# A routing tail reordered: pad addresses ahead of places, five pad scatters behind the first rows' low part, fewer filler matmuls

## The reference

```python
def reference(**kw):                                     # B, H, S, D = 4, 8, 768, 48
    attn_out = _attn_ref(r, k, v, w, u)                  # decayed linear attention, per head 48 x 48 state
    x = attn_out.transpose(0, 2, 1, 3).reshape(3072, 384)
    gate = 1.0 / (1.0 + np.exp(-(x @ w_gate)))           # 384 -> 1536
    x = gate * (x @ w_val) @ w_out                       # 1536 -> 384
    xn, en = x / (norm(x) + 1e-6), emb / (norm(emb) + 1e-6)
    logits = xn @ en.T / tau                             # 8 experts
    expert_idx = np.argmax(logits, axis=1)
    gate_w = softmax(logits)[np.arange(N), expert_idx]
    for e in range(8):
        mask = expert_idx == e
        out[mask] = gate_w[mask, None] * (np.maximum(x[mask] @ w1[e], 0.0) @ w2[e])   # 384 -> 1024 -> 384
    return out
```

## Time and profile before

| | |
|---|---|
| runs | 866.97 us median, 865.52 to 870.53 |
| profiled execution | 868.17 us, its span 866.4 us |
| PE busy | 835.3 us, 96% of the span |
| DVE, ACT, POOL busy | 448.5, 297.5, 415.4 us |
| mean granted TensorE clock | 0.976 |
| DMA | 82.02 MB, mean 95 GB/s |

### The profile page before, as it was taken

The page is one execution under the profiler, slowest core; times in us unless marked ns, Lnnn a source line. Parts: engine busy times, 40 slices in busy tenths (PEclk is TensorE's granted clock), DMA queues, the critical chain, the costliest instruction groups (busy, mean ns, idle before and its releaser), DMA issues.

```text
span 866.4 us, 20325 instructions
## 1 busy us (share of the span) xinstructions
PE 835.3 (96%) x7442; PEld 789.6 (91%) x7443; DVE 448.5 (52%) x1057; ACT 297.5 (34%) x610; POOL 415.4 (48%) x446
## 2 busy tenths in 40 slices
PE   5999899999999999999999999989999999999995
PEld 5899899999999999999999999978999999989995
DVE  7579555455455455355455451485267277267100
ACT  1134322322232232232232233514444544444442
POOL 4346245435436436426427413254566566466444
PEclk8599999999999999999999999999999999999999
DMA  9643413203202302302302200236345344344110
GB/s 281 219 125 123 132 35 97 68 29 87 85 28 85 86 26 79 95 20 85 95 19 86 88 20 10 74 128 178 96 140 161 100 146 147 107 155 142 45 36 29
DMA packets 78420, 82.02 MB, mean 95 GB/s; under 512 B 5816, under 2 KB 75648, under 8 KB 78352
## 3 DMA queue, kind: packets, MB, share of 16 engines
q1 hardware_dynamic: 65200, 60.29, 23.2%
q10 hardware_dynamic: 9216, 9.55, 3.8%
q0 software_dynamic: 3936, 11.23, 3.5%
HBM read 69.83 MB, written 12.01 MB: 94 GB/s over the span
## 4 chain that ended last, share of the span: by engine, by line
PE 93%; DVE 4%; issue 1%; POOL 1%; DMA 0%; ACT 0%; SPq 0%; POOLq 0%; ACTq 0%; DVEq 0%
PE ps L1340 34%; PE ps L1361 18%; PE ps L1443 14%; PE ps L1428 13%; PE ps L1451 3%; PE ps L1286 2%; PE ps L1263 2%; PE ps L1383 2%; PE ps L1294 1%; PE ps L1270 1%; PE ps L1300 1%; PE ps L1408 1%; DVE weights L1125 1%; PE ps L1310 1%; DMA w_col<-in_w 0%
## 5 line engine op out<-in xcount | busy, mean ns | idle before, releaser
L1340 PE MATMUL ps<-x_groups,weights 128*128 128x384 f32 x1728 | 319.5, 341 | 0.2 <-DVE weights L1125 0.2
L1340 PEld LDWEIGHTS ps<-x_groups,weights 128*128 128x128 f32 x1728 | 301.1, 190 | 2.6 <-issue 0.5
L614 POOL TENSOR_TENSOR hT<-gate,hT 128x384 fp32r<-128x384 f32 x96 | 104.5, 1091 | 144.7 <-ACT hT L743 144.7
L1361 PE MATMUL ps<-weights,hT 128*128 128x392 f32 x864 | 160.6, 344 | 0.0
L1361 PEld LDWEIGHTS ps<-weights,hT 128*128 128x128 f32 x864 | 152.6, 188 | 0.4
L1443 PE MATMUL ps<-weights,hT 128*128 x672 | 124.2, 339 | 1.7 <-ACT h_f L851 1.7
L1428 PE MATMUL ps<-weights,x_groups 128*128 (+1 forms) x504 | 122.8, 397 | 1.2 <-issue 1.2
L1082 DVE TENSOR_TENSOR gate<-ps,gate 128x384 f32<-128x384 f32 x96 | 53.5, 557 | 126.3 <-PE ps L1340 119.7
L1443 PEld LDWEIGHTS ps<-weights,hT 128*128 128x128 f32 x672 | 115.9, 188 | 1.9 <-issue 1.9
L1428 PEld LDWEIGHTS ps<-weights,x_groups 128*128 128x128 f32 x504 | 92.6, 188 | 20.4 <-issue 1.7
L1068 DVE CAST weights<-staged 128x768 fp32r<-128x768 f32 x56 | 49.0, 874 | 93.1 <-PE ps L1428 54.8
(11 more groups left out here) (179 smaller groups left out, 970.7 us busy)
## 6 DMA issues: line engine op xcount, KB each, us to landing
staged<-in_moe_w SPq DMA_DIRECT2D x60, 384.0 KB
r_in<-routed ACTq DMA_DIRECT2D x30, 192.5 KB
rk_raw<-in_rt SPq DMA_DIRECT2D x21, 256.0 KB, 3.6
rk_raw<-in_kt SPq DMA_DIRECT2D x21, 256.0 KB, 4.1
r_in<-in_r SPq DMA_DIRECT2D x21, 192.0 KB, 2.4
k_in<-in_k SPq DMA_DIRECT2D x21, 192.0 KB, 2.5
v_in<-in_v SPq DMA_DIRECT2D x21, 192.0 KB, 2.3
A_room<-in_v_swap SPq DMA_DIRECT2D x21, 96.0 KB, 2.7
```

What stands on the lines that cost most here:

```text
L614: g.tensor_tensor(hT_lo[:, f, :], gate[:, f % 2, :], hT_hi[:, f, :].bitcast(F32), ALU.subtract).then_inc(hlo_ready, 1)
L1340: ins = te.matmul(ps[:, bank[f % 2], 0:GT], wt[:, c, fs], x[:, half, c, :], start=(c == 0 and m == 0), stop=(c == KC - 1 and m == 2))
L1361: ins = te.matmul(ps[:, BX2[i], 0:XW], h[:, f, ts], wt[:, f, :], start=(f == 0 and m == 0), stop=(f == FC - 1 and m == 2))
```

## The change

It does four things. In `weigh` two small DVE instructions (the cast of the token number and its increment) now stand that stood in `scale`; in `scale` the token's copy into the row comes first and the scaled row last, with `rows_ready` on it, and `choose` waits for that. In `put` of the last tile the two instructions that make the pads' addresses come before those that make the rows' places. On POOL pads 2 to 5 go from before `keep_tokens(0)` and `rows_lo(0)` to behind them, in front of pads 6 and 7 (five pads, 2 to 6, count to `pads_out`, as before). On PE the fillers go from 36 and 14 to 32 and 4.

```diff
--- before.py
+++ after.py
@@ -655,8 +655,6 @@
                 pad(0, first_pad)
                 scatter(G, half, 2)
                 pad(1, second_pad)
-                for e in range(2, E - 2):
-                    pad(e, pads_out)
 
             for i in range(TPG):
                 for stage in range(STAGES):
@@ -709,7 +707,8 @@
 
             keep_tokens(0)
             rows_lo(0)
-            pad(E - 2, pads_out)
+            for e in range(2, E - 1):
+                pad(e, pads_out)
 
             pad(E - 1, stored)
             def finish(last):
@@ -999,6 +998,8 @@
                 T = G * TPG + i
                 logits = x2[:, DM:XW]
                 dve.wait_ge(x2_psum, T + 1)
+                if T > 0:
+                    dve.wait_ge(rows_ready, T)
                 ve.tensor_copy(x2[:, :], ps[:, BX2[i], 0:XW]).then_inc(x2_copied, 1)
                 dve.wait_ge(x2_copied, T + 2)
                 ve.tensor_reduce(top[:, i, 0:1], logits, AX_X, ALU.max).then_inc(route_step, 1)
@@ -1020,24 +1021,28 @@
                 dve.wait_ge(route_step, T * 9 + 5)
                 ve.scalar_tensor_tensor(out=top[:, i, 4:5], in0=top[:, i, 0:1], scalar=-1.0, in1=top[:, i, 3:4],
                                         op0=ALU.mult, op1=ALU.mult).then_inc(bias_ready, 1)
+                ve.tensor_copy(token_i[:, :], token[:, :]).then_inc(route_step, 1)
+                dve.wait_ge(route_step, T * 9 + 6)
+                ve.tensor_scalar(token[:, :], token[:, :], float(P), None, ALU.add).then_inc(route_step, 1)
 
             def scale(G, half, i):
 
                 T = G * TPG + i
                 buf = (half * TPG + i) % 2
+                dve.wait_ge(route_step, T * 9 + 7)
+                ve.tensor_copy(row[:, buf, DM:ROW].bitcast(I32), token_i[:, :])
                 dve.wait_ge(probs_ready, T + 1)
                 ve.tensor_scalar(top[:, i, 5:6], top[:, i, 5:6], 1e-9, None, ALU.add).then_inc(route_step, 1)
-                dve.wait_ge(route_step, T * 9 + 6)
+                dve.wait_ge(route_step, T * 9 + 8)
                 ve.reciprocal(top[:, i, 6:7], top[:, i, 5:6]).then_inc(route_step, 1)
-                dve.wait_ge(route_step, T * 9 + 7)
-                ve.tensor_scalar(row[:, buf, 0:DM], x2[:, 0:DM], top[:, i, 6:7], None, ALU.mult)
-                ve.tensor_copy(token_i[:, :], token[:, :]).then_inc(route_step, 1)
-                dve.wait_ge(route_step, T * 9 + 8)
-                ve.tensor_copy(row[:, buf, DM:ROW].bitcast(I32), token_i[:, :])
-                ve.tensor_scalar(token[:, :], token[:, :], float(P), None, ALU.add).then_inc(route_step, 1)
-
                 dve.wait_ge(route_step, T * 9 + 9)
-                dve.sem_inc(rows_ready, 1)
+                ve.tensor_scalar(row[:, buf, 0:DM], x2[:, 0:DM], top[:, i, 6:7], None, ALU.mult).then_inc(rows_ready, 1)
+
+            def pads():
+
+                ve.tensor_scalar(pad_at[:, :], filled[:, :], lane[:, 0:1], None, ALU.add).then_inc(pad_step, 1)
+                dve.wait_ge(pad_step, 1)
+                ve.tensor_copy(pad_i[:, :], pad_at[:, :]).then_inc(pads_ready, 1)
 
             def put(b, G, half, i):
 
@@ -1050,6 +1055,8 @@
                 ve.tensor_tensor(place_m[:, :], place[:, :], chosen[:, i, :], ALU.mult).then_inc(place_step, 1)
                 ve.tensor_tensor(filled[:, :], ranks[:, E:2 * E], filled[:, :], ALU.add).then_inc(place_step, 1)
                 dve.wait_ge(place_step, T * 4 + 3)
+                if T == NT - 1:
+                    pads()
                 ve.tensor_reduce(pos[:, buf, :], place_m[:, :], AX_X, ALU.add).then_inc(place_step, 1)
                 dve.wait_ge(place_step, T * 4 + 4)
                 dve.wait_ge(scattered[buf], (b * TPG + ((half * TPG + i) // 2 + 1)) * 16)
@@ -1112,11 +1119,6 @@
                     put(b, G, half, 2)
                 else:
                     put(b, G, half, 2)
-
-                    dve.wait_ge(place_step, (G * TPG + 2) * 4 + 3)
-                    ve.tensor_scalar(pad_at[:, :], filled[:, :], lane[:, 0:1], None, ALU.add).then_inc(pad_step, 1)
-                    dve.wait_ge(pad_step, 1)
-                    ve.tensor_copy(pad_i[:, :], pad_at[:, :]).then_inc(pads_ready, 1)
                     scale(G, half, 2)
 
             def make_lo(kind, j):
@@ -1461,9 +1463,9 @@
                 if first:
                     pe.wait_ge(plan, 4)
 
-            keep_clock(BT, 36)
+            keep_clock(BT, 32)
             turn_rows(0)
-            keep_clock(BT, 14)
+            keep_clock(BT, 4)
             run_slots(pe, slot, output)
```

## The result

The changed kernel takes 873.31 us (median of 7 runs, 872.47 to 875.72); the kernel before, on the same chip, 868.87 us (7 runs, 865.52 to 870.53). The ratio is 1.0064, 95% interval 1.0052 to 1.0076: slower by more than the 0.5% that a measurement of this kernel can tell from no change. The forecast was 867.2 in a range of 864.6 to 869.8.

A forecast was written before the change was run, and what follows sets the result against it. PE, holding 93% of the chain, was taken to bound the kernel, measured at slot 0's output start. Terms of -0.1 and +0.3 for the clock summed to +0.2, giving 867.2 us on the median, range 864.6 to 869.8.

The forecast's parts named there:

- the moved pads: POOL, behind slot 0's low part: six pads instead of two delay load 2, so output starts at 599.5, before 599.60.
- A: Start of ACT's first copy of slot 0's rows after the transposes: from 585.22 to 583.6, bounds 584.9 and 582.0.
- rival (a): The gain gets through if the 1.39 before ACT's copy was pad traffic: output at 597.2, 864.6 us; chance 0.22 with (e).
- The last pad's landing: Before ACT's load 2: landing 1.85 later by the quiet row, more beside traffic; load 2 at A + 11.6 to 12.5.
- Load 2's flight and what follows: From load 2 to slot 0's output: flight 3.0 to 4.26, then transposes 0.33; output at A + 14.9 to 17.1.
- The clock: PE's new pauses inside `hidden(1)` and before slot 2's rows may lower the clock: bounds 0 and 1.6, 0.3 taken.
- The fillers: PE around slot 0's transposes: with 8 records left behind them, `hidden(0)` starts at 584.1 instead of 587.99, 3.9 us earlier.
- the point by which I measured: Start of slot 0's output matmuls on PE, 599.60 before; every us it moves moves the end by one us.
- Rival (b): The moved pads cost more than the earlier start brings: output at 600.9, 868.3 us, 869.9 with low clock; chance 0.12.
- (c): Fewer fillers and PE's two new pauses lower the clock in the output matmuls: 1.6 instead of 0.3, 868.5 us; chance 0.08.
- (d): The pads delay expert 1's weights so that PE waits for them: a few us, 872 and more; chance 0.03.
- (e): Only the fillers act and the pads hide: `hidden(0)` and all behind it 2.4 earlier, 864.6 us; chance 0.22 with (a).

The follow-up runs named there:

- experiment 9: The changed kernel with expert 1's weight loads held back until all pads have landed; 870.57 us against 867.16 for the kernel before, ratio 1.0036.
- experiment 4: The changed kernel with the old 36 and 14 fillers; 872.9 us against 867.69 for the kernel before, ratio 1.0066.
- experiment 12: The changed kernel with slot 1 written out on PE and 16 fillers in the wait for load 2; 872.53 us against 866.44 for the kernel before, ratio 1.0071.
- experiment 3: The kernel before with only the fillers changed, 32 and 4 instead of 36 and 14; 867.58 us against 867.69, ratio 0.9999.
- experiment 5: The changed kernel with load 2 waiting for pad 2 alone, pads 3 to 6 awaited before load 3; 868.98 us against 865.35 before, ratio 1.0043.
- experiment 7: The kernel of experiment 6 with fillers 10 and 1 of 512 columns for 32 and 4 of 128; 868.92 us against 865.35 before, ratio 1.0044.
- experiment 6: The changed kernel with load 2 waiting for pad 2 alone and pads 5 to 7 behind slot 1's low part; 866.57 us against 865.35, ratio 1.0000.
- experiment 8: The changed kernel with pads 2 and 3 put back ahead of the first rows; 871.78 us against 865.35 for the kernel before, ratio 1.0073.
- experiment 1: The changed kernel with pads 2 to 5 put back ahead of the first rows; 867.76 us against 867.69 for the kernel before, ratio 0.9995.
- experiment 10: The kernel of experiment 6 with pad 2 ahead of the first rows; 864.47 us against 867.16 for the kernel before, ratio 0.9967.
- experiment 2: The kernel before with only the pads moved; 873.11 us against 867.69, ratio 1.0063.
- experiment 11: The kernel of experiment 10 with fillers 12 and 1 of 512 columns for 32 and 4 of 128; 864.09 us against 867.16 before, ratio 0.9962.

## Why the prediction was wrong

The step that failed is the moved pads, which were said to give back just what the earlier start brings: a start of the output at A + 15.9 = 599.5. It was 604.14, 4.64 later, and this is made of three terms.

- **A itself, 0.77.** Forecast 583.6, measured 584.37. Several errors lie in it. DVE brought 0.05 instead of 0.3: the copy out of PSUM, forecast at 570.25, began at 570.52, as in the kernel before. Load 0 went at 580.95, not 578.7: from the last scatter's issue to load 0 it took 4.73 us where I took the 2.83 of the kernel before (579.02 - 576.19) for fixed. The transposes took 0.91 at the low clock instead of 0.55. Against that, the flight was even shorter (2.48 to the transposes, not 3.0), and the 1.39 between the transposes' end and ACT's copy, which I kept, was gone: 0.03. Here rival (a)'s premise was right: in the runs with pads 2 to 5 ahead the delay was 1.39, 0.43 and 2.77, and each time ACT began 1.42 to 1.55 us after pad 5's issue ended; with at most two of them ahead it was 0.03 or 0.04.
- **The last pad's landing, 1.6.** Forecast load 2 at A + 11.6 to 12.5, measured A + 13.65. The pads' pitch was right, the last issue began at A + 8.59. But I took the landing of a pad from a quiet row, 1.85 behind the issue's end, and let it reach some 2.7 beside traffic. It was 3.3 (4.27 - 0.98), and another 0.8 went by to load 2's issue (0.3 taken). The Trainium skill, DMA: Bandwidth & Descriptors, Queues, rings and completion order, says that all queues share 16 engines, which I used to argue that load 2 gains; it holds for the pads themselves as well, which experiment 9 shows: with the weights held back the landing is 2.0 (2.98 - 0.98).
- **Load 2's flight and what follows, 2.27.** Forecast 3.3 to 4.6, taken as 3.85; measured 4.27 + 0.55 + 1.30 = 6.12. I had no term for the 1.30: before, PE reached the output without waiting and the row "issue" was not there. Everywhere that PE waited for slot 2's rows, 0.9 to 1.6 of issue followed.

The clock was the fourth term: 0.3 taken, 3.02 in the profiled execution. The bound of 1.6 came from a stretch of 3.2 us at the low clock; here it was low for over 6. Experiments 4 and 12 say that this is not what the typical loss consists of.

**The fillers.** `hidden(0)` began 2.3 earlier, at 585.69 (forecast 584.1, 3.9 earlier), and this was rightly said to be away from the point by which I measured. The pause inside `hidden(1)`, forecast at 2, was 0.36, since `hidden(1)` itself began at 593.13 and not at 591. Not foreseen: the seam then loses the clock in `hidden(0)` (4.65 here, 5.97 in experiment 3).

**The rivals.** Rival (b) was the true one, with its place and point of decision right, and its price too low: 600.9 for the output's start against 604.14. It had the output at A + 16.4, and it came at A + 19.8. What I held against it, that pads at a pitch of 1.28 are paced by POOL, is true of the issues (0.98 to 1.01 each, gaps of 0.30) and not of the landings. And it named only the wait for the landings; POOL's copy behind the pads, which the prediction had ready at about A + 11.4 and did not count among load 2's conditions, holds load 2 as well once that wait is gone (experiment 5). (c) did happen in the profile, together with (b). (d) did not: PE never waited for weights, and DVE's casts waited for PE longer than before (63.6 against 54.8). (a) and (e) fell.

**The chances.** 0.94 for "same" was the second fault. The rivals' bounds were each made as if the others stood at their middle, so none but (d), which did not happen, went past 869.9; late scatter, late landing, issue and clock all lie the same way and come from one thing, a seam whose transfers now stand in PE's chain. The mark named for a wrong prediction (the output more than 1.5 from 599.6) is the one that showed it.

**What stays open.** Why ACT's copy stumbles while pads are in flight; why experiment 7 is slower than 6; why four pads cost as much as six (experiment 8); and why four of the five kernels of one chip lose more than their seams show.

## What to carry to other kernels

Before moving small transfers out of one wait, list every wait that counts their landings, and everything that stands behind them on the issuing engine: here the next load waited for all five, and its other condition, a POOL copy, stood behind them too. Price a landing by one beside the same traffic, not by a quiet one (here 3.3 in the change against 1.85). What gained was to give the next load the one pad that it needs and issue that pad early, with the rest behind everything that PE waits for.

## What the runs showed of the hardware

**An instruction fetch that falls on a transfer goes with its late completion.** From the start of the last scatter's issue to load 0 it took 4.6 to 5.3 us in some kernels and 2.8 to 3.1 in others. The DMA queues of the changed kernel from 578.2 to 580.9, while ACT waited for that scatter:

```profile
q0 software_dynamic: 89, 0.22, 23.1%
q8 instruction: 1, 0.02, 3.0%
```

One packet of instructions holds one of the 16 engines for 0.030 x 16 x 2.7 = 1.3 us. Where it began 1.2 to 2.1 us behind the start of the scatter's issue (the change, experiments 1, 4, 9, 10, 12) the scatter was late; where 2.3 us or more (before, 2, 3, 5, 6, 8), it was not. In the kernel before it came at 579.75, beside load 0, whose last 9 packets were late; 144 packets shared evenly over 16 engines are 9 for each. The prediction put those down to the pads; in experiments 1 and 3, with the same four pads beside load 0 but the fetch ahead of it, the transposes began 2.74 after load 0's issue, not 4.26. The fetch fits as the cause, the pads do not. The one test of it is a pair: experiment 11 differs from 10 in PE's fillers alone, which are longer and so fewer instructions. The fetch, which must then be PE's, moved from 577.1 to 592.6, and the scatter's time to load 0 fell from 4.58 to 2.88. (In experiment 7 it moved too, to 590.85, but there the scatter had not been late.) No run shows by what way it delays the scatter.

**A pad among weights.** From the start of its issue to the waiting load it took 3.8 us with the weights held back and up to 8.0 beside them (584.19 to 592.21, experiment 6), and the issue itself 1.5 to 1.7 instead of 0.98 for some (experiments 2, 5, 6 and 8).

**PE's issue behind a wait.** After a wait for rows, the output matmuls of a slot start 0.94 to 1.63 us behind the transposes, mostly 1.27 to 1.30; with PE kept busy in the wait by fillers (experiment 12) it is 0.69, without a wait 0 to 0.36. In the code PE reads the slot's table values there; whether these cost the time was not tried.

**The clock.** Idle for 3.9 and 4.15 us, PE then ran at the lower level (0.50); with 0.47 of wait ahead of the transposes and 1.29 behind them (experiment 4) it stayed at the higher one for the output. Short waits are not safe by that: with 0.50 and 1.27 at the same places, and 1.96 of wait inside `hidden(1)` ahead of them, the output took 6.03 (experiment 5), and with 0.70 and 1.63 it took 6.02 (experiment 6), each with a granted clock of 0.50 in one stretch of 2 us.
